# Two weight pairs and the first heads' splits change between GpSimd and VectorE in the attention part of a three-stage kernel

## The reference

```python
scores = q @ k.transpose(0, 1, 3, 2) / sqrt(64)          # q, k, v: (4, 8, 576, 64)
rel = pos[:, None] - pos[None, :]
scores = where((rel >= 0) & (rel < 128), scores - slope[h] * abs(rel), -1e9)
attn = softmax(scores)                                   # over keys; sum + 1e-9
x = (attn @ v), heads side by side                       # (2304, 512)
h = x @ moe_w_in;   x = (h * sigmoid(1.702 * h)) @ moe_w_out      # d_ff 2048
h = x @ moe2_w_in;  out = where(h >= 1, h, where(h <= -1, 0, (h + 1)**2 / 4)) @ moe2_w_out
```

## The kernel before

| work | engine | place |
|---|---|---|
| adds, splits of weight pair 0 | POOL | after heads 11, 12, 13 and 14, 15, 16 |
| adds, splits of weight pair 1 | POOL | after heads 17, 18, 19 and 20, 21, 22 |
| adds of weight pair 2 | POOL | after heads 23, 24, 27 |
| splits of x's operands A11, S1, S2, A12 | POOL | after heads 25, 26, 28, 29 |
| sums S1, S2 | VectorE | behind the bias of steps 57 and 64 |
| rounding A11, S1, S2, A12, S3, S4 | ACT | steps 55, 58, 65, 66, 77, 79 |

## Time and profile before

### The profile page before, as it was taken

How to read it: one execution, slowest core, us unless ns; L and a number is a source line. 1 busy time by engine, 2 the same in 40 slices (tenths; PEclk the granted TensorE clock), 3 DMA queues, 4 the chain that set the end, 5 groups by cost and what they waited for, 6 DMA issues and landing times.

```text
span 876.9 us, 15508 instructions
## 1 busy us (share of the span) xinstructions
PE 853.5 (97%) x5746; PEld 846.3 (97%) x5746; DVE 703.6 (80%) x973; ACT 536.5 (61%) x788; POOL 127.3 (15%) x90
## 2 busy tenths in 40 slices
PE   6998889999999999999999999999999999999998
PEld 6998889999999999999999999999999999999998
DVE  5887786567798887677997988888989789889784
ACT  4776767567675555676744546766556466765431
POOL 3789988100000000000000000000000000000000
PEclk9999999999999999999999999999999999999999
DMA  9999872268856464487857564489555643888822
GB/s 206 238 255 232 232 201 82 98 227 316 289 193 239 169 251 148 188 305 286 298 180 276 186 222 166 159 288 330 187 204 190 235 177 145 284 284 296 310 76 73
DMA packets 63369, 191.17 MB, mean 218 GB/s; under 512 B 7488, under 2 KB 14400, under 8 KB 59456
## 3 DMA queue, kind: packets, MB, share of 16 engines
q1 hardware_dynamic: 63296, 190.18, 64.7%
HBM read 117.81 MB, written 72.35 MB: 217 GB/s over the span
## 4 chain that ended last, share of the span: by engine, by line
PE 86%; POOL 7%; DVE 3%; issue 1%; ACT 1%; SPq 1%; DMA 1%; POOLq 0%; ACTq 0%; DVEq 0%
PE ps L1037 79%; POOL qk_hi L881 3%; POOL k_lo L878 2%; PE ps L1005 2%; PE ps L971 2%; PE ps L984 1%; POOL w_first L901 1%; DVE qk_hi L1503 1%; DMA qk_raw<-qkT 1%; DVE probs L1523 1%; SPq L566 1%; ACT w_first L1243 1%; PE ps L999 1%; DVE wst L1555 0%; PE ps L1014 0%
## 5 line engine op out<-in xcount | busy, mean ns | idle before, releaser
L1037 PE MATMUL ps<-arena,w_first 128*128 128x384 f32 x1764 | 331.6, 336 | 0.9 <-ACT ps L1284 0.9
L1037 PEld LDWEIGHTS ps<-arena,w_first 128*128 128x128 f32 x1764 | 310.7, 188 | 2.4 <-issue 1.7
L1037 PE MATMUL ps<-arena,w_rest 128*128 128x384 f32 x1260 | 240.8, 337 | 0.9 <-ACT ps L1284 0.8
L1037 PEld LDWEIGHTS ps<-arena,w_rest 128*128 128x128 f32 x1260 | 220.1, 188 | 2.0 <-issue 1.7
L1611 DVE TENSOR_TENSOR arena<-raw_first,arena 128x768 fp32r<-128x768 f32 (+1 forms) x114 | 148.7, 1318 | 78.2 <-ACT arena L1256 78.2
L1256 ACT ACTIVATE arena<-raw_first 128x768 fp32r<-128x768 f32 (+1 forms) x120 | 132.0, 1117 | 45.5 <-DVE raw_first L1577 38.8
L1037 PE MATMUL ps<-w_rest,arena 128*128 128x256 f32 x945 | 132.4, 281 | 0.0
L1037 PEld LDWEIGHTS ps<-w_rest,arena 128*128 128x128 f32 x945 | 121.1, 189 | 0.1
L1037 PE MATMUL ps<-w_first,arena 128*128 128x256 f32 x567 | 88.0, 282 | 0.0
L1611 DVE TENSOR_TENSOR arena<-raw_rest,arena 128x1536 fp32r<-128x1536 f32 (+1 forms) x48 | 71.3, 1486 | 12.4 <-ACT arena L1256 12.3
L1037 PEld LDWEIGHTS ps<-w_first,arena 128*128 128x128 f32 x567 | 76.0, 189 | 0.0
(11 more groups left out here) (111 smaller groups left out, 977.8 us busy)
## 6 DMA issues: line engine op xcount, KB each, us to landing
gd<-g SPq DMA_DIRECT2D x24, 1536.0 KB, 6.1
raw_rest<-gd SPq DMA_DIRECT2D x32, 768.0 KB, 5.1
qk_raw<-qkT SPq DMA_DIRECT2D x60, 288.0 KB, 5.7
wst<-w_pairs SPq DMA_DIRECT2D x32, 512.0 KB, 6.5
raw_first<-gd SPq DMA_DIRECT2D x16, 768.0 KB, 5.9
yd<-ust SPq DMA_DIRECT2D x6, 1536.0 KB, 6.3
wd<-ust SPq DMA_DIRECT2D x4, 1536.0 KB, 9.1
raw_first<-yd SPq DMA_DIRECT2D x4, 1536.0 KB, 7.3
```

Of the source, the lines that this page charges most:

```text
L1037: last = nc.tensor.matmul(to, stationary, moving, start=start and n == 0, stop=n == len(steps) - 1, skip_group_check=True)
```

## The change

Weight pair 1 is summed and split on VectorE, weight pair 2 summed there. The second part of head 0 is split by VectorE, the first keys of head 1 by POOL, the queries of heads 2 and 3 by VectorE right behind their casts. Head 4's cast comes one step earlier. S1's sum moves from step 57 to 58 (from position 2 to 3), S2's from 64 to 63 (4 to 3), and ACT's roundings of x's operands shift by a step at three places.

The new `split_rest_keys` makes k_lo of head 1's second piece, VectorE's `split_rest` the keys and the queries of head 0's; `split_weights_part` takes 256 columns in its step 0 and three operands of 256 each in steps 1 and 2.

```diff
+DVE_QUERIES = (2, 3)
...
         def load_operands(head):
...
-                sp.wait_ge(first_split[slot], 2)
+                sp.wait_ge(first_split[slot], 2 - slot)
+            if head - SPLIT_RING == 1:
+                sp.wait_ge(first_keys_split, 1)
...
     def _(pool):
-        def split_rest(e):
...
+        def split_first_keys():
+            pool.wait_ge(first_rounded, 2)
+            nc.gpsimd.tensor_tensor(piece_lo(1, True), piece_keys(qk_raw, 1, True), f32(piece_keys(qk_hi, 1, True)),
+                                    ALU.subtract).then_inc(first_keys_split, 1)
...
+        def split_rest_keys():
+            pool.wait_ge(rest_rounded, 2)
...
         def split_head(head):
...
-            pool.wait_ge(qk_split[slot], splits(head) - 1)
-            nc.gpsimd.tensor_tensor(all_queries(qk_hi, head), ...)
+            if head not in DVE_QUERIES:
+                pool.wait_ge(qk_split[slot], splits(head) - 1)
+                nc.gpsimd.tensor_tensor(all_queries(qk_hi, head), ...)
...
-        split_rest(0)
-        split_rest(1)
+        split_first_keys()
+        split_rest_keys()
...
-            if head in (17, 18, 19):
-                add_weights(1, head - 17)
-            if head in (20, 21, 22):
-                split_weights(1, head - 20)
-            if head in (23, 24, 27):
-                add_weights(2, (23, 24, 27).index(head))
...
     def _(act):
-            if m in (55, 58, 65, 66, 77, 79):
+            if m in (55, 59, 64, 65, 77, 79):
...
     def _(dve):
         def round_first(e):
...
+            if e == 0:
                 nc.vector.tensor_tensor(piece_lo(e, True), ...).then_inc(first_split[e], 1)
...
+        def split_rest():
+            dve.wait_ge(rest_rounded, 1)
...
         def round_head(head):
...
+            if head in DVE_QUERIES:
+                dve.wait_ge(qk_rounded, head - 1)
+                nc.vector.tensor_tensor(all_queries(qk_hi, head), all_queries(qk_raw, head), f32(all_queries(qk_hi, head)),
+                                        ALU.subtract).then_inc(qk_split[slot], 1)
...
+        def split_weights_part(w, step):
+            dve.wait_ge(w_rounded, 2 * nth(w) + (1 if step == 0 else 2))
...
+            nc.vector.tensor_tensor(to, a, f32(hi), ALU.subtract).then_inc(w_ready, 1)
...
             if m == 0:
                 round_first(1)
+                split_rest()
...
-            if m in (57, 64):
-                sum_operand(0, S1 if m == 57 else S2)
+            if m == 43:
+                add_weights(1)
+            if m in (46, 48, 51):
+                split_weights_part(1, (46, 48, 51).index(m))
+            if m in (58, 63):
+                sum_operand(0, S1 if m == 58 else S2)
+            if m == 66:
+                add_weights(2)
             for head in range(SPLIT_RING, 2 * PAIR_COUNT):
-                if m == last_use(head - SPLIT_RING) + CAST_LAG[head % 2]:
+                if m == last_use(head - SPLIT_RING) + (1 if head == SPLIT_RING else CAST_LAG[head % 2]):
```

More of the change, by code:

```diff
@@ L174, in build @@
     first_split = [sem(f"first_split{e}") for e in range(2)]
+    first_keys_split = sem("first_keys_split")
     rest_rounded = sem("rest_rounded")
@@ L879, in split_head @@
                                     ALU.subtract).then_inc(qk_split[slot], 1)
-            pool.wait_ge(qk_split[slot], splits(head) - 1)
-            nc.gpsimd.tensor_tensor(all_queries(qk_hi, head), all_queries(qk_raw, head), f32(all_queries(qk_hi, head)),
-                                    ALU.subtract).then_inc(qk_split[slot], 1)
+            if head not in DVE_QUERIES:
+                pool.wait_ge(qk_split[slot], splits(head) - 1)
+                nc.gpsimd.tensor_tensor(all_queries(qk_hi, head), all_queries(qk_raw, head), f32(all_queries(qk_hi, head)),
+                                        ALU.subtract).then_inc(qk_split[slot], 1)
             pool.wait_ge(qk_split[slot], splits(head))
@@ L951, in scores @@
             if q == 0:
-                if d in (2, 4):
-                    pe.wait_ge(first_split[0 if d == 2 else 1], 2)
+                if d == 2:
+                    pe.wait_ge(first_split[0], 2)
+                elif d == 4:
+                    pe.wait_ge(first_split[1], 1)
+                    pe.wait_ge(first_keys_split, 1)
                 elif d == 3:
@@ L1272, in _ @@
                 round_both((30, 45, 70).index(m))
-            if m in (55, 58, 65, 66, 77, 79):
-                round_operand(0, (55, 58, 65, 66, 77, 79).index(m))
+            if m in (55, 59, 64, 65, 77, 79):
+                round_operand(0, (55, 59, 64, 65, 77, 79).index(m))
         def seed_b(D, n):
@@ L1562, in split_weights @@
             nc.vector.tensor_tensor(rest[:, :, 1], w_others(w), f32(rest[:, :, 0]), ALU.subtract).then_inc(w_ready, 2)
+        def split_weights_part(w, step):
+            dve.wait_ge(w_rounded, 2 * nth(w) + (1 if step == 0 else 2))
+            if step == 0:
+                to, a, hi = made_first(w)[:, 1], w_b11(w), made_first(w)[:, 0]
+            else:
+                some = slice(3 * step - 3, 3 * step)
+                to, a, hi = made_rest(w)[:, some, 1], w_others(w)[:, some], made_rest(w)[:, some, 0]
+            nc.vector.tensor_tensor(to, a, f32(hi), ALU.subtract).then_inc(w_ready, 1)
         def sum_operand(k, i):
```

21 lines of the change are left out of this document (11 added, 10 removed).

## The result

The changed kernel takes 882.58 us (median of 20 runs, 880.3 to 884.87), the kernel before 880.14 (20 runs, 879.06 to 882.14): a ratio of 1.0024, interval 1.0016 to 1.0032, so 2.4 us slower, and within the 0.3% that the forecast called no change. The profiled execution took 883.84 us, its span 882.1; it stands 5.1 us above the profiled one of before and 1.3 above its own median, so two profiles put side by side show about twice the difference of the medians.

What follows compares the result with a forecast made beforehand. Feed-forward matmuls, 79% of the chain, stay untouched; attention turns are bound by TensorE at 8.07 us, with waits for a backlogged POOL. Terms sum to +2.5 us: 882.6 on the median's scale, named 882.0, range 873.5 to 886.5.

Steps and rivals of the forecast that it cites:

- Start: First heads: queries on VectorE beside k_lo on POOL and head 4's earlier cast win 1.9 us by step 11.
- Turn 8: Steps 40 to 45: second pair's adds at step 43 delay the pair transposition 2.8 us, 1.6 more if the clock falls.
- Turn 9: Second pair's splits at steps 46 and 48; the second waits for head 21's k_lo on POOL, +1.7 us.
- Turn 10: Last split of the second pair on VectorE at position 1, +0.2 us.
- Turn 11: POOL's backlog and the clock's fall end, but S1's sum at position 3 meets head 25's k_lo; -2.7 us.
- Turn 12: S2's sum at step 63 waits for POOL's S1 split ahead of the pair's write; +1.1 us.
- Turn 13: Third pair's adds at step 66 wait between POOL's splits, delaying the transposition; +1.3 us, the wait covering the clock's fall.
- turns 14 and 15: The wait for head 31 stays, A12's split being in its way as before; 0 us.
- Rival A: Attention turns: the port costs little, since POOL freed of 12 us leaves it open; 873 us, chance 0.38.
- Rival B: Turns 8 and 13: TensorE waits for VectorE's adds and the clock falls; 886.4 us, chance 0.15.
- Rival C: POOL's backlog stays because it waits for casts anyway, and turn 11's wait returns; 885 us, chance 0.05.
- "same" (0.27): Outcome for the whole kernel: measured time from 877.5 to 882.7 us, not told from no change; chance 0.27.

Runs made afterwards that it cites:

- the spread kernel: Changed kernel with VectorE's pieces spread one to a step and the first pair's splits also on VectorE; 875.38 us, ratio 0.9951 to before.
- experiment 4: Changed kernel with the second pair's three adds back on POOL, its splits left on VectorE; 879.70 us, ratio 1.0002 to before.
- experiment 5: Changed kernel with POOL's two splits for head 19 cut to 8 columns, leaving most of its rests out of the result; 881.26 us, ratio 1.0014.
- experiment 7: Changed kernel with the third pair's adds back on POOL, after heads 23, 24 and 27; 882.47 us, ratio 1.0023 to before.
- experiment 6: Changed kernel with the second pair's three adds moved from step 43 to behind the copy of the pair's tail in step 44; 881.66 us, ratio 1.0017.
- Experiment 3: Changed kernel with S1's and S2's sums back in steps 57 and 64, ScalarE's rounding with them; 880.77 us, ratio 1.0007 to before.
- experiment 8: The spread kernel: changed kernel with VectorE's pieces one to a step, plus the first pair's splits on VectorE; 875.38 us, ratio 0.9951 to before.
- experiment 11: The spread kernel with POOL's S1 split behind head 27, S2's sum at step 69, third pair's adds at 66, 71, 73; 871.81 us, ratio 0.9908 to before.

## Why the prediction was right, point by point

The time (882.58 for 882.0) and the two signs, start won and moves lost, came out. The terms in order:

*Start, -1.9.* Measured -1.6, alone (878.50 for 880.14; 1.4 against the runs beside it), under the spread kernel (875.38 for 876.97), and as the earlier start of turn 4. In the six profiles with this start and a clock of 1.00 all through it, turn 4 begins at 42.90 to 43.33, against 44.90 to 45.04 with the old one: 1.6 to 2.1 us, about what the sum has. In the other five, the changed kernel's among them (0.83 from 10 to 20 us), the clock fell in the start; in the three with the old start it did not. Step 11 was forecast at 27.4; its scores begin at 27.64. The mechanism is in the timeline: queries on VectorE begin 0.1 us before k_lo on POOL, the later one holds the wait (1.92 for 1.42), and TensorE waits for the exponentials instead of POOL, against the earlier trace rows.

```profile
17.10 0.76 DVE L1519 TENSOR_TENSOR qk_hi<-qk_raw,qk_hi 64x576 fp32r<-64x576 f32 x1
17.21 1.92 POOL L884 TENSOR_TENSOR k_lo<-qk_raw,qk_hi 128x576 fp32r<-128x576 f32 x1 [1.29 <-DVE qk_hi L1516]
...
20.73 0.44 PE L988 MATMUL ps<-ident,probs 128*128 128x128 f32 x2 [0.71 <-ACT probs L1194]
```

*Turn 8, +2.8, and +1.6 with the clock.* The adds were to last 3.1 us from first to last end and lasted 2.97; without a fall of the clock the turn would be 8.07 + 2.87 + 2.64 = 13.58 (both waits with the 0.25 that modelled ends hide), for the forecast 13.8. The waiter was named wrong: it is the weighing of values in step 45, which reuses what the pair's write reads, one group before the pair transposition. The clock was taken as a rival at 0.15, and it came: 16.18 - 13.58 = 2.6 us, which takes the turn to +5.2, just over the high bound with the clock (+5.0). Taking the adds away gives 2.9 of the median back (experiment 4), freeing the port alone 1.3 (5).

*Turn 9, +1.7.* Measured +2.6, beyond the bound of +2.2. The split at step 48 waited for POOL less than thought (it lasted 1.22 us, not 1.9) and TensorE 0.65; so the turn's own part is 8.07 + 0.90 = 8.97, 0.5 above before. The other 2.1 us of 11.12 are the lower clock carried over from turn 8. So the cause in this profile is another than the term's. That the mechanism exists is shown by experiments 4, 5 and 7, where turn 9 ran at a clock of 1.00: TensorE waited 1.56, 1.56 and 1.57 us for heads_out, and the turn took 9.85, 9.86 and 9.86, +1.4 for the forecast +1.7; and by experiment 6, where the same split took 2.04.

*Turn 10, +0.2*, measured 0.0. *Turn 11, -2.7*, measured -2.8 (9.77 for the forecast 9.85): the backlog ended, and S1's sum at position 3 cost 1.48 us of wait. Experiment 3 gives the sum's move 1.1 of it.

*Turn 12, +1.1.* Measured +1.7, just over the bound of +1.6: VectorE idle 1.36 us for S1's split (forecast 1.1), TensorE 3.16 for 2.52, and 1.0 of lower clock. These rows show the chain:

```profile
126.82 2.23 POOL L924 TENSOR_TENSOR arena<-raw_first,arena 128x768 fp32r<-128x768 f32 x1
...
129.16 2.19 DVE L1604 TENSOR_TENSOR raw_first<-raw_first 128x768 f32<-128x768 f32 x1 [1.36 <-POOL arena L924]
...
137.66 3.40 DVE L1572 TENSOR_TENSOR wst<-wst 128x512 f32<-128x512 f32 x3
```

*Turn 13, +1.3*, the term that failed: -0.1. The third pair's adds did stretch to 3.40 us, but they stand at position 1, and TensorE waited for nothing in this turn. It ran on the lower clock, as it did before; the forecast had the wait cover the clock, and in fact the slower TensorE covered the adds. The mechanism itself is in other profiles: in experiments 4, 5 and 6 the same adds stretched to 3.74, 4.33 and 4.90 us, and TensorE waited 0.97, 0.82 and 0.97 us for heads_out in this turn. It took 10.41, 10.72 and 10.74 us, at mean clocks of 0.91, 0.84 and 1.00. Experiment 7 can't price it, since POOL's extra work made turn 12 longer.

Term by term the misses in the profiled execution are start +0.3, turn 8 +2.4, turn 9 +0.9, turns 10 and 11 -0.2, turn 12 +0.6, turn 13 -1.4, turns 14 and 15 -0.1, together +2.5; the attention's last pair transposition starts 5.0 us later (161.80 for 156.79), just inside the bound of 162. The medians differ by 2.4, since the profiled execution lies 1.3 above its median and that of before 1.4 below. So the forecast of the median owes something to misses that cancel. How much of the clock's part the median holds can be bounded from the runs' mean clocks: 0.991 for the changed kernel, 0.993 for before. The unrounded difference, 0.0024 of 880 us, is 2.1 us of TensorE's work, an estimate and an upper one, since a slower TensorE also covers waits, as in turn 13. The sum has a gain of 1.6 from the clock in turn 11 and no loss elsewhere; the runs have a loss of up to 2.1. The time came out in spite of this: the forecast took the clock's fall away and did not put it back, and that is luck.

Rival A (the port costs little) is refuted by experiment 5. Rival B had the right mechanism for turn 8, and for turn 13 not in the changed kernel's profile. Rival C is refuted by POOL's busy time in turns 9 and 10 and by turn 11, where no wait for POOL is left. The range was said to take in A's time, but its low end of 873.5 lies above A's 873; and "same" (0.27), which came, had the least chance of the three outcomes. None of the rivals had the reading that experiments 8 and 11 gave: VectorE's total work was not what made the changed kernel's turns long. In the fastest kernel VectorE carries three splits more than in the changed one, and its turns 8 to 10 are 9.33, 8.54 and 9.08, with one or two pieces in each.

## What to carry to other kernels

When work moves to an engine with time to spare, its place in that engine's queue counts before its length: ask for each piece what stands behind it and who waits for that. Single instructions in several steps, at a fifth step behind the last copy that TensorE needs, instead of three in a row in front of the pair's write, with three splits more on VectorE and one operand's split later on POOL, turned +2.4 us into -8.3. Part of that is the clock, which stayed up where the long waits were gone. So price an idle time of TensorE with the lower clock behind it, as a range, and look at the mean clock of every run before reading a profile.
